# The first batch of an attention taken by pairs of heads, six tokens to a partition, with x's k-tiles made from the transposed bank and the first weight slots split by parts

## The reference

```python
# batch, n_heads, seq, head_dim = (4, 8, 576, 64); tokens 2304, d_model 512
kv = np.einsum('bhsd,bhse->bhde', k, v)
out = np.einsum('bhsd,bhde->bhse', q, kv)
rms = np.sqrt(np.mean(out * out, axis=-1, keepdims=True) + 1e-06)
x = (out / rms * g_norm)            # then heads side by side: [2304, 512]
...
g = x @ w_gate                      # 512 x 1536
silu = g * (1.0 / (1.0 + np.exp(-g)))
x = silu * (x @ w_val) @ w_out      # 512 x 1536, 1536 x 512
...
h = x @ w_in                        # 512 x 2048
g = np.maximum(h, 0.0) + np.log1p(np.exp(-np.abs(h)))
return g @ w_out                    # 2048 x 512
```

## Time and profile before

| | us |
|---|---|
| median of 3 runs | 914.52 (913.83 to 914.61) |
| the profiled execution | 912.8, of which 911.0 are the span from the first instruction to the last |
| PE busy in the span | 896.5 |
| DVE, ACT, POOL busy | 524.8, 348.1, 76.0 |
| start of step 1 on PE (gate) | 34.18 |
| start of step 4 on PE (gate) | 53.02 |

### The profile page before, as it was taken

How to read it: one execution, slowest core, us unless ns; L and a number is a source line. 1 busy time by engine, 2 the same in 40 slices (tenths; PEclk the granted TensorE clock), 3 DMA queues, 4 the chain that set the end, 5 groups by cost and what they waited for, 6 DMA issues and landing times.

```text
span 911.0 us, 13266 instructions
## 1 busy us (share of the span) xinstructions
PE 896.5 (98%) x5128; PEld 849.2 (93%) x5128; DVE 524.8 (58%) x1009; ACT 348.1 (38%) x603; POOL 76.0 (8%) x34
## 2 busy tenths in 40 slices
PE   6899999999999999999999999999999999999998
PEld 5799999999999999999999998998999998998997
DVE  2645642454245323223333888878878878878875
ACT  1425340333033301000233654644654554644653
POOL 2444300000000000000354000000000000000000
PEclk9999999999999999999999999999999999999999
DMA  9794261035111200000134000000000000000000
GB/s 225 176 207 132 72 126 53 24 81 105 54 29 41 79 4 1 1 1 1 49 118 135 24 1 1 35 0 0 35 0 0 35 0 0 35 0 0 36 1 35
DMA packets 84201, 44.38 MB, mean 49 GB/s; under 512 B 40768, under 2 KB 76736, under 8 KB 84160
## 3 DMA queue, kind: packets, MB, share of 16 engines
q1 hardware_dynamic: 84000, 43.80, 18.4%
q10 hardware_dynamic: 160, 0.00, 0.0%
HBM read 35.52 MB, written 8.26 MB: 48 GB/s over the span
## 4 chain that ended last, share of the span: by engine, by line
PE 97%; DVE 1%; SPq 1%; DMA 1%; ACT 0%; issue 0%; ACTq 0%
PE bank L544 24%; PE bank L545 24%; PE bank L546 24%; PE bank L615 7%; PE bank L616 7%; PE bank L614 7%; PE bank L482 2%; PE bank L467 1%; DMA v<-in_v 1%; SPq L296 0%; DVE sums L820 0%; DVE x_norm L829 0%; DVE x_lo L848 0%; DVE x_hi L846 0%; SPq L364 0%; DVE q_t L783 0%
## 5 line engine op out<-in xcount | busy, mean ns | idle before, releaser
L544 PE MATMUL bank<-x_hi,arena 128*128 128x384 f32 x960 | 322.9, 336 | 2.0 <-DVE x_lo L848 1.9
L546 PE MATMUL bank<-x_hi,arena 128*128 128x384 f32 x960 | 321.9, 335 | 0.0
L545 PE MATMUL bank<-x_lo,arena 128*128 128x384 f32 x960 | 321.3, 335 | 0.0
L544 PEld LDWEIGHTS bank<-x_hi,arena 128*128 128x128 f32 x960 | 180.2, 188 | 7.5 <-DVE x_lo L848 2.1
L545 PEld LDWEIGHTS bank<-x_lo,arena 128*128 128x128 f32 x960 | 180.2, 188 | 3.8
L546 PEld LDWEIGHTS bank<-x_hi,arena 128*128 128x128 f32 x960 | 180.1, 188 | 0.0
L884 DVE TENSOR_TENSOR act_a<-act_a,bank 128x384 f32<-128x384 f32 x72 | 39.8, 553 | 230.1 <-PE bank L546 224.5
L698 ACT ACTIVATE act_a<-bank 128x384 f32<-128x384 f32 x72 | 35.3, 490 | 231.7 <-PE bank L546 231.6
L718 ACT ACTIVATE act_a<-bank 128x384 f32<-128x384 f32 x96 | 47.3, 493 | 178.9 <-PE bank L546 178.7
L616 PE MATMUL bank<-arena,g_lo 128*128 128x512 f32 x288 | 113.8, 395 | 0.0
L615 PE MATMUL bank<-arena,g_hi 128*128 128x512 f32 x288 | 113.6, 394 | 0.0
(11 more groups left out here) (56 smaller groups left out, 789.3 us busy)
## 6 DMA issues: line engine op xcount, KB each, us to landing
stage<-in_moe_w_out SPq DMA_DIRECT2D x28, 256.0 KB, 3.7
out_dram<-out_stage SPq DMA_DIRECT2D x18, 256.0 KB, 2.1
k<-in_k SPq DMA_DIRECT2D x16, 256.0 KB, 2.9
v<-in_v SPq DMA_DIRECT2D x16, 256.0 KB, 3.3
stage<-in_moe_w_in SPq DMA_DIRECT2D x16, 256.0 KB, 2.6
xy<-in_q SPq DMA_DIRECT2D x48, 72.0 KB, 3.0
stage<-in_moe_w_gate SPq DMA_DIRECT2D x12, 256.0 KB, 3.3
stage<-in_moe_w_val SPq DMA_DIRECT2D x12, 256.0 KB, 3.6
```

Source lines behind the costliest of these rows:

```text
L544: nc.tensor.matmul(ps, hi, rhs_hi, start=first, stop=False)
L545: nc.tensor.matmul(ps, hi, rhs_lo, start=False, stop=False)
L546: return nc.tensor.matmul(ps, lo, rhs_hi, start=False, stop=last)
```

## The change

**The layout.** Batch 0 is loaded by pairs of heads: for each pair one load of q, one of k, one of v, 96 partitions with six tokens each (`J0`, `P0`), 1536 bytes in a run. For K'V the order of tokens doesn't matter as long as k and v agree. For q it does: POOL puts the six tokens' rows of two heads side by side (`q_rows0`), PE transposes each of the six 96x128 blocks into two banks, and ACT's two copies scatter them so that tokens are in order again.

**The order.** For pair t: K'V, fill of one block, q*KV for the first three tiles (384 tokens), square, sum, root, normalise, three transposes. The transposed bank is k-tile t of x as it is: ACT writes x_hi from it with the gain as a scale, DVE writes x_lo. `xy` isn't used for these tokens. Tiles 3 and 4 are made later (`late_q_times_kv` in steps 0 and 1, their roots after silu(1), transposes at the end of step 2, stores at step 3).

**The weights.** Slots 0 and 1 are rounded and subtracted by parts of 512 elements, in the order of HIGH_ORDER and LOW_ORDER, and gate and val of steps 0 to 2 take all products with the high weights first (`high_products`) and those with the low weights behind (`low_products`). Slots 0 and 1 are loaded behind all of q, k and v. SP's load of slot 2 waits for w_out's part of slot 0. Ten products with zeros (IDLE_PRODUCTS) stand at PE's front.

```diff
+J0 = 6
+P0 = S // J0
+X_NEEDED = [0] + [n - LATE0 for n in (NT + 2, 2 * NT, 2 * NT + 3, 3 * NT + 2, 4 * NT)]
+IDLE_PRODUCTS = (7, 3)
+HIGH_ORDER = [("val", 0), ("gate", 1), ("out", 0), ("val", 1), ("out", 1)]
+LOW_ORDER = [("gate", 0), ("val", 0), ("gate", 1), ("out", 0), ("val", 1), ("out", 1)]
...
+        def load_first(t):
+            for src, n in ((q, "q"), (k, "k"), (v, "v")):
+                sp.dma_start(heads0[t][n][:, :, :, :].rearrange("p h j d -> p h (j d)"),
+                             src[0, 2 * t:2 * t + 2, :, :].rearrange("h (p j) d -> p h (j d)", j=J0)
+                             ).then_inc(first_q_loaded[t] if n == "q" else first_kv_loaded[t], 16)
...
         def load_step1(f):
             if f >= 2:
-                sp.wait_ge(w_ready, f - 1)
+                sp.wait_ge(w_ready, low_count(f - 2))
...
-        for j in range(1, NT - 2):
-            load_q(0, j, q_tiles0[j], first_q_loaded[j])
+            load_first(t)
         load_step1(0)
-        for j in range(NT - 2, NT):
-            load_q(0, j, q_tiles0[j], first_q_loaded[j])
         load_step1(1)
+        sp.wait_ge(qt0_done, KT)
         load_step1(2)
...
+        for t in range(KT):
+            pool.wait_ge(first_q_loaded[t], 16)
+            if t >= 2:
+                pool.wait_ge(qt0_done, t - 1)
+            nc.gpsimd.tensor_copy(q_rows0[t % 2][:, :, :].rearrange("p j (h d) -> p j h d", h=2),
+                                  heads0[t]["q"][:, :, :, :].rearrange("p h j d -> p j h d")).then_inc(q_rows_ready, 1)
+        pool.wait_ge(part_loaded["gate", 0], 16)
+        nc.gpsimd.tensor_copy(part1(0, 0, "gate"), stage1[:, 0, 0:DM]).then_inc(w_hi_first, 1)
...
+        for what, f in LOW_ORDER[1:]:
+            low_part(f, what)
+        for f in range(2, NF1):
+            low(high_count(f), arena[:, f * SLOT1:(f + 1) * SLOT1], stage1[:, f % 2, :], RAW1)
...
+        pe.wait_ge(zeros_ready, 3)
+        idle_products(IDLE_PRODUCTS[0])
+        pe.wait_ge(const_ready, 1)
+        first_transpose_q(0)
+        idle_products(IDLE_PRODUCTS[1])
         for t in range(KT):
+            first_kv_product(t)
+            first_q_times_kv(t)
+            if t + 1 < KT:
+                first_transpose_q(t + 1)
+            if t:
+                first_transpose_x(t - 1)
...
+        def up1_first():
+            pe.wait_ge(w_hi_first, 1)
+            for t in range(KT - 1):
+                pe.wait_ge(xs_ready, t + 1)
+                high_products(gate_ps, 0, "gate", [t])
+            pe.wait_ge(w_ready, low_count(0, "gate"))
+            low_products(gate_ps, 0, "gate", range(KT - 1))
+            late_q_times_kv(LATE0)
+            first_transpose_x(KT - 1)
+            pe.wait_ge(w_hi_ready, high_count(0, "val"))
+            high_products(val_ps, 0, "val", range(KT - 1))
+            pe.wait_ge(w_ready, low_count(0, "val"))
+            low_products(val_ps, 0, "val", range(KT - 1))
+            pe.wait_ge(xs_ready, KT)
+            products(gate_ps, 0, "gate", KT - 1).then_inc(gate_done, 1)
+            products(val_ps, 0, "val", KT - 1).then_inc(val_done, 1)
...
+        def first_x_high(t):
+            act.wait_ge(xt0_done, t + 1)
+            nc.scalar.activation(x_hi[:, t, :], xt_ps0[:, 0:CH], ACT.Copy, scale=gain[:, 0:1]).then_inc(xs_hi_ready, 1)
...
+        for t in range(KT - 1):
+            first_square(t)
+            first_copy_q(t + 1, 0)
+            first_root(t)
+            first_copy_q(t + 1, 1)
+            if t:
+                first_x_high(t - 1)
+        first_square(KT - 1)
+        first_x_high(KT - 2)
+        first_root(KT - 1)
...
-        split_high(1)
+        part_high(0, "val")
+        nc.scalar.preload_act_table_set("silu_and_others")
+        first_x_high(KT - 1)
+        part_high(1, "gate")
+        part_high(0, "out")
         silu(0)
-        store_x(NT - 2, xt_ps0[(NT - 2) % 2])
+        part_high(1, "val")
+        part_high(1, "out")
+        square_up(-LATE0, LATE0, late_ps[0], square_late[0])
         split_high(2)
...
+        for t in range(KT):
+            if t >= 2:
+                first_x_low(t - 2)
+            first_fill(t)
+            if t:
+                first_normalize(t - 1)
+            first_sum(t)
+        first_x_low(KT - 2)
+        first_normalize(KT - 1)
+        first_x_low(KT - 1)
```

More of the change, by code:

```diff
@@ new lines, in products @@
+        def products(ps, f, what, t):
+            return passes(ps[:, 0:CH], w1(f, 0, what, t), w1(f, 1, what, t), x_hi[:, t, :], x_lo[:, t, :],
+                          t == 0, t == KT - 1)
+        def up1_first():
[14 more added lines that the diff above has]
+            products(val_ps, 0, "val", KT - 1).then_inc(val_done, 1)
```

375 lines of the change are left out of this document (228 added, 147 removed).

## The result

The changed kernel takes 921.92 us (median of 4 runs, 921.54 to 924.38) where the kernel before takes 914.19 on the same chip: a ratio of 1.009, 95% interval 1.0072 to 1.0108. That is 7.7 us slower, outside the range of the prediction (912.3 to 918.9).

A forecast was written before the change was run, and what follows sets the result against it. PE bounds the kernel, with weights just in time. Step 4 at 28.5 + 25.6 = 54.1 instead of 53.02 adds 1.1 us to the profiled 912.8, giving 913.9; 1.7 more to the median gives 915.6, range 912.3 to 918.9.

The forecast's parts named there:

- The chain behind L0: SP's loads of slots 2 to 4, then slot 4's rounding and subtraction: step 4 can't start before L0 + 25.6 us.
- L0: Time when slot 0's last part (w_out's) is subtracted, releasing slot 2's loads: forecast 28.5 us; later than 27.4 means slower.
- PE's own path: PE's work up to step 4: step 1 at 27.8 instead of 34.18, 4.4 us won net, 5.9 lost waiting for weights.
- the entry: Kernel start to the first q*KV, priced at PE's lower clock: first q*KV at 9.2 us.
- the exit: From q*KV of pair 3 to w_out's subtraction of slot 0: 8.3 us.
- from round 0 on: PE's clock in the rounds of pairs: at the upper level after the entry; a round costs 5.1 us if not.
- rival B: Clock stays down in the rounds: two further rounds +1.0 us each, exit 0.6, so 918.2 us; chance 0.12.
- The loads aren't the bound of this loop: Rounds of pairs: 3.54 MB of loads end at about 18 us; K'V of pair 3 comes at 17.7.
- The loop: Round through four engines, from q*KV to the fills: 4.07 us each, two of them, q*KV of pair 3 at 20.2.
- POOL's copy: In the entry, POOL's new copy of 768 elements of q: 0.75 us, bounds 0.5 and 1.5.
- rival C: Entry or SP's chain longer: POOL's copy +0.75 us, DMA backlog up to 0.5 twice, 917.4 us; chance 0.16.
- what follows it is the same work on both sides: Everything after the start of step 4: same work before and after the change, with PE the bound.

The follow-up runs named there:

- e1: Changed kernel with ten idle products instead of three behind the first transposes of q; ratio 1.0056 to the kernel before.
- e2: e1 plus 2, 4, 5 and 5 idle products between K'V and q*KV of the four pairs; ratio 1.0039 to the kernel before.
- e4: Changed kernel with SP waiting for q of pair 0 to land before issuing pair 1's loads; ratio 1.0057 to the kernel before.
- e5: Changed kernel with no idle products at all; ratio 1.0082 to the kernel before.
- e6: e2 with ACT's copies of q written contiguously instead of at every sixth place (output not the reference's); ratio 1.0040 to the kernel before.
- e3: Changed kernel with SP issuing batch 1's eight k and v loads ahead of slot 2's loads; ratio 1.0070 to the kernel before.
- e11: Kernel before with 8 idle products ahead of its first K'V and 3 ahead of each later one of batch 0; ratio 1.0014 to the kernel before.
- e7: e2, e3 and e4 together, five idle products ahead of K'V 0, slot 0's w_out ahead of slot 1's w_gate; ratio 0.9984 to the kernel before.
- e10: e7 with 7 idle products in all instead of 28 (0, 2, 2 and 3 in the rounds); ratio 1.0031 to the kernel before.
- e9: e7 with three idle products ahead of K'V 0, slot 2 loaded part by part, slot 3 rounded before the late tiles' roots; ratio 1.0001 to the kernel before.

## Why the prediction was wrong

**The chain behind L0 was right as a mechanism and in its sum, and the sum was in part luck.** L0 + 25.6 was forecast, and 60.43 - 34.38 = 26.05 measured; slot 2 was issued 0.1 us behind L0. Piece by piece: slot 2 and the k/v loads took 7.7 (34.47 to 42.21) for 6.45, slot 3's and the eight of q 8.0 (to 50.25) for 6.96, slot 4's loads until ACT could start 5.05 (to 55.30) for 7.08; the rest was as forecast. The issues were 2.3 us longer, the landing 2.0 shorter. In e1, e2, e4, e5 and e6, with the same queue, the chain is 24.7 to 26.2. PE waits 1.4 us for the low parts in step 2 and 3.1 for slot 3; the forecast had 1.8 for slot 2's, and 1.1 and 2.1 for slots 3 and 4. The whole of slots 3 and 4 came at slot 3. PE's own path came out much later than forecast (step 1 at 33.41 for 27.8), but the chain was the longer one all the same. e3 confirms that these issues are the chain. The price of a late L0 was also known: break-even at 27.4.

**L0 itself was wrong: 28.5 forecast, 34.4 measured.** These 5.9 us are the miss. They split as follows, by one trace each, so to some tenths.

*The clock, 3.5 us (e2 against the changed kernel): 0.5 at the entry, 1.1 in each of the rounds to pairs 1 and 2, nothing in the last, 0.8 in the exit.* This is the step that failed: the prediction put PE at the upper level "from round 0 on" and held that "that it falls again between the rounds is less likely", citing a window in which PE was busy 1.23 of 2.00 and the products behind ran at the full rate. It was rival B, chance 0.12, and priced too low (1.0 a round, 0.6 for the exit, 2.6 in all). Two things went past me. The first was a gap that I had not seen, 2 us of no work ahead of K'V 0; the idle products at the front had raised the clock, as the prediction says they would, and it was lost there. And the window that I cited lay in a stretch where the work behind it was dense; it was no evidence on rounds with holes. The Trainium skill (TensorE: Matmul & The Clock Gate, The HAM clock gate) makes the lower level the idle state, released by activity. The traces agree with both halves: with idle products across the gap (e1) the first K'V took 0.92, and without (changed, e3) 1.50 and 1.55.

*The loads, about 0.9 us.* "The loads aren't the bound of this loop" was the second sentence that failed. I compared their end (18 us; measured 19.0) with the last K'V, not each pair's landing with its own K'V. The entry has a term for the landing of q alone, 3.1 us behind its issue, and none for v of pair 0, which landed 6.4 behind its own: entry at 9.8 with the clock up (e2), 0.6 later than the 9.2. v of pair 1 landed at 11.54, and K'V 1 waited 0.3 for it. (What the lower level added to the entry, 9.8 to 10.35, is in the 3.5 above, though the forecast had already reckoned with it there: it priced work on PE where PE waited for data.) e4 shows that the order of issue was at fault and not the volume.

*e2's own idle products, 0.4 us.* They held the second q*KV from 13.02 to 13.43. In the changed kernel, which has none there, this belongs to the clock's share, as far as one can tell. With the two above the round to pair 1 is 3.6 us in e2, where 2.85 was forecast; in e1, without wait or idle products in it, it is 3.16.

*The loop, 0.5 us.* At the upper clock the two further rounds took 4.27 and 4.38 for 4.07. The chain through the engines is the one that was written down: in e2's trace of 13.43 to 17.70, q*KV until ACT's square 0.87, square 0.52, sum 0.59, root 0.20, copy 0.46, x_hi 0.57, x_lo 0.54, fills 0.52. The copy had been put at 0.32, since no row showed a write at a stride of six.

*The exit, 0.5 us.* 8.8 with the clock up, for 8.3.

3.5 + 0.9 + 0.4 + 0.5 + 0.5 = 5.8, and rounding is the rest. POOL's copy was right (0.82 for 0.75), so rival C's first part did not happen. Its second did: the issues behind L0 were 2.3 us longer, and only the quicker landing of slot 4 kept the chain within 0.45 of the forecast.

**What lay outside the prediction.** The 0.9 us at 506 us is in none of its terms: "what follows it is the same work on both sides" is true of the work, not of the place at which PE's code is fetched.

So the forecast's form (PE's head gains, SP's chain gives it back, one time L0 decides) stands. On its own terms the changed kernel should have been at 913.9 + 5.9 + 0.4 + 0.9 = 921.1 in the profiled execution, which took 921.95. Of the 0.8 that is left, 0.6 lies outside the span: 2.4 to 2.6 us in every execution of a kernel with the new head and 1.7 to 1.8 with the old (e11's too). It is in none of the terms either, and its cause is open.

## What to carry to other kernels

Where loads are issued back to back, cost each one's landing by its place in the stream (bytes ahead of it by the measured GB/s, and what moves beside it), and set it against its own consumer, not the last landing against the last consumer. Where a head has gaps of a microsecond or two on PE, price it at both levels of the clock and look at the gaps first; a few products that do nothing, where PE waits anyway, are a cheap test, and here they were worth 3.5 us of the head. See that they end before the data is there: in e1 and e7 they lasted past it and took some back. When a wait on a shared queue decides, list what else stands in that queue and needn't: eight issues moved ahead of the wait and one part of a slot read out first, with the first loads held back and idle products in the rounds, turned a loss of 0.9% into a gain of 0.16%, and the late tiles' sum and normalizations taken earlier on DVE, with slot 2 loaded part by part, made it 0.3%. No one of them does it: e10 has all four with most idle products taken out, and loses 0.3%. The one move that wasn't checked against who waits for the moved step (e9) took 2 us back.
